# Three of the first four weight pieces loaded behind the first tile's inverse: a delta-rule attention with two feed-forward blocks on one core

## The reference

```
k_n = k / (norm(k) + 1e-6);  state = 0
for t in range(768):
    y[t]  = q[t] @ state
    state = state + beta[t] * outer(k_n[t], v[t] - state^T k_n[t])
```

```
x   = relu(x @ w_in)**2 @ w_out                      # 384 -> 2048 -> 384
out = max(x @ w1, x @ w2, x @ w3) @ w_out2           # 384 -> 768 -> 384
```

## Time and profile before

| what | value |
| --- | --- |
| median of 3 timed runs | 949.91 us (947.35 to 950.4) |
| the profiled execution's own time | 946.07 us |
| its span | 944.1 us |
| TensorE busy | 868.9 us, 92% of the span |
| VectorE, ScalarE, GpSimd busy | 45%, 28%, 30% |
| mean granted clock of TensorE | 0.969 of full speed |

### The profile page before, as it was taken

The page is one execution under the profiler, slowest core; times in us unless marked ns, Lnnn a source line. Parts: engine busy times, 40 slices in busy tenths (PEclk is TensorE's granted clock), DMA queues, the critical chain, the costliest instruction groups (busy, mean ns, idle before and its releaser), DMA issues.

```text
span 944.1 us, 20905 instructions
## 1 busy us (share of the span) xinstructions
PE 868.9 (92%) x9148; PEld 743.6 (79%) x9148; DVE 428.9 (45%) x641; ACT 265.8 (28%) x464; POOL 285.4 (30%) x392
## 2 busy tenths in 40 slices
PE   2326699999999999999999999999999999999998
PEld 2326588878888888888888888887898989898988
DVE  6936365574566456645544444434323232323231
ACT  2211343233223322332233233633222222122221
POOL 4147898813941394139400000721000000000000
PEclk8658899999999999999999999999999999999999
DMA  7976764165424532353223134012020202010000
GB/s 185 220 142 148 160 148 102 52 138 132 106 60 97 131 105 60 93 129 80 64 63 91 36 95 123 9 51 67 1 67 1 67 1 67 0 67 1 34 1 34
DMA packets 123435, 76.27 MB, mean 81 GB/s; under 512 B 94320, under 2 KB 107120, under 8 KB 123344
## 3 DMA queue, kind: packets, MB, share of 16 engines
q1 hardware_dynamic: 121088, 73.89, 31.7%
q10 hardware_dynamic: 2256, 1.05, 0.4%
HBM read 53.18 MB, written 20.45 MB: 78 GB/s over the span
## 4 chain that ended last, share of the span: by engine, by line
PE 89%; DMA 3%; DVE 3%; SPq 3%; issue 1%; ACT 0%; ACTq 0%; DVEq 0%
PE psum L71 25%; PE psum L73 24%; PE psum L72 24%; PE psum L667 3%; PE psum L605 2%; PE psum L591 2%; PE psum L616 2%; PE psum L655 2%; PE psum L674 2%; PE psum L631 1%; PE psum L642 1%; DMA dram_f<-sol_f 1%; SPq L372 1%; DMA kz_first<-in_kT 1%; SPq L326 1%
## 5 line engine op out<-in xcount | busy, mean ns | idle before, releaser
L967 DVE TENSOR_TENSOR sq<-relu 128x512 f32<-128x512 f32 x96 | 76.2, 793 | 151.2 <-ACT relu L1103 151.1
L73 PE MATMUL psum<-x_lo,wb 128*128 128x512 f32 x324 | 126.3, 390 | 0.0
L72 PE MATMUL psum<-x_hi,wb 128*128 128x512 f32 x324 | 126.3, 390 | 0.0
L71 PE MATMUL psum<-x_hi,wb 128*128 128x512 f32 x324 | 126.2, 389 | 0.0
L71 PE MATMUL psum<-x_hi,win 128*128 128x512 f32 x288 | 116.3, 404 | 9.0 <-DVE x_lo L956 7.9
L1103 ACT ACTIVATE relu<-psum 128x512 f32<-128x512 f32 x96 | 57.3, 597 | 228.6 <-PE psum L73 228.6
L104 POOL TENSOR_TENSOR sol_tmp<-sol_b,sol_f 128x31 f32<-128x31 f32 (+15 forms) x155 | 90.1, 581 | 84.6 <-DMA sol_b<-dram_b 72.7
L71 PE MATMUL psum<-sq_hi,wout 128*128 128x512 f32 x288 | 114.2, 396 | 1.0 <-DVE sq_lo L972 1.0
L72 PE MATMUL psum<-x_hi,win 128*128 128x512 f32 x288 | 113.2, 393 | 0.0
L73 PE MATMUL psum<-x_lo,win 128*128 128x512 f32 x288 | 113.1, 393 | 0.0
L73 PE MATMUL psum<-sq_lo,wout 128*128 128x512 f32 x288 | 112.4, 390 | 0.0
(11 more groups left out here) (99 smaller groups left out, 1280.0 us busy)
## 6 DMA issues: line engine op xcount, KB each, us to landing
kz<-in_kT SPq DMA_DIRECT2D x40, 192.0 KB, 3.5
v_t<-in_vn SPq DMA_DIRECT2D x12, 384.0 KB, 3.5
qa<-in_qT SPq DMA_DIRECT2D x24, 192.0 KB, 3.8
nz<-in_kn SPq DMA_DIRECT2D x24, 192.0 KB, 4.3
x2T<-x SPq DMA_DIRECT2D x6, 768.0 KB, 4.1
x_raw<-x2T SPq DMA_DIRECT2D x6, 768.0 KB, 4.6
out_dram<-o_t SPq DMA_DIRECT2D x24, 192.0 KB, 1.9
raw_wb<-in_w SPq DMA_DIRECT2D x18, 192.0 KB, 4.4
```

Source lines behind the costliest of these rows:

```text
L71: nc.tensor.matmul(out, lhs_hi, rhs_hi, start=first, stop=False)
L72: nc.tensor.matmul(out, lhs_lo, rhs_hi, start=False, stop=False)
L73: return nc.tensor.matmul(out, lhs_hi, rhs_lo, start=False, stop=last)
L967: nc.vector.tensor_tensor(d.sq[:], d.relu[:], d.relu[:], ALU.mult).then_inc(s.sq_ready, 1)
```

## The change

In SyncE's list the loads of piece 1 and piece 2, which stood right behind that of piece 0, now stand behind the store of tile 0's inverse and the loads of f1 and fz of chunk 0. The load of piece 4, with its wait for the fourth Gram product (kk_done), moves from ahead of that store to behind the loads of pieces 1 and 2. Piece 0 stays.

```
@@ -412,20 +412,20 @@
             sp.wait_ge(s.nz_zero, 1)
             load_kn(0)
             load_piece(0)
-            load_piece(1)
-            load_piece(2)
             sp.wait_ge(s.qk_done, 1)
             load_k(1, True)
             load_v(1)
             sp.dma_start(rows_of[2][:], kn[2]).then_inc(s.rows_in2, 16)
             sp.wait_ge(s.ob_zero, 3)
             load_ob(0)
-            sp.wait_ge(s.kk_done, 4)
-            load_piece(4)
             sp.wait_ge(s.fz_zero, 1)
             store_f(0)
             load_f1(0)
             load_fz(0, [1])
+            load_piece(1)
+            load_piece(2)
+            sp.wait_ge(s.kk_done, 4)
+            load_piece(4)
             for c in (2, 3):
                 sp.wait_ge(s.cg_ready, c + 1)
                 store_blocks(c, BLOCKS, s.b_stored)
```

## The result

The changed kernel took 953.88 us (median of 16 runs, 951.59 to 955.46), the one before 949.70 (16 runs, 945.15 to 952.12). The ratio is 1.005 with a 95% interval of 1.0035 to 1.0064: 3.3 to 6.1 us slower. A second comparison gave 953.40 against 950.23, ratio 1.0034 (1.0017 to 1.005), 3.2 us slower. The forecast was 953.8 and slower.

The account below looks back on a forecast made before the run. Until 104.3 us a chain of waits through the inverse's store and tile 1's root was taken as the bound, then TensorE. Root +3.6 and held norms +0.3 gave +3.9 on the 949.91 median: 953.8 us, range 949.1 to 957.2.

Parts of the forecast that it names:

- the text's own signs of being wrong: Root below 60.5, first dense matmul not moved as far as the root, or end not as far as that matmul.
- The store, the pieces and the root: Tile 1's root on ScalarE: store lands at 48.6, piece 2 is split at 61.0, root at 61.9 instead of 58.33, +3.6 us.
- the two cases: Piece 2 landing behind piece 1: 3.9 us in one earlier pair of loads, 4.9 in another; the middle, 4.4, was taken.
- VectorE beside GpSimd: Tile 1's norms held by GpSimd's low halves of piece 2, one or two meetings: +0.3 us, bounds -0.6 and +1.9.
- The cover: GpSimd's low halves, clearing sol_f, piece 4's issue and ScalarE's fz loads would be hidden under other waits, costing nothing.
- Pieces at peak rate: Rival: piece 2 lands 2.1 us behind piece 1, root at 59.6, sum +1.6, 951.5 us, no difference; chance 0.18.
- Piece 4 in the way of piece 2: Rival: piece 4's loads interleave with piece 2, landing up to 4 us later; root 65.9, +7.9, 957.8 us; chance 0.13.
- The faster side: Rival: the inverse's store sets the chain, so the root comes up to 8.8 us earlier; 941.1 us; chance 0.05.

Follow-up runs that it names:

- the kernel in which GpSimd waits: Changed kernel, with GpSimd waiting for the norms of tile 1 before making the low half of piece 2; 951.61 against 951.19 us before, ratio 1.0009.
- the kernels with the root first: Changed kernel, with ScalarE taking fz loads and tile 1's root before splitting pieces 1 and 2: 0.9944; splits later still: 0.9961; piece 4 also behind piece 3: 0.9924.

## Why the prediction was right, and where only by luck

The path was right: the root of tile 1 is released by the later of the store and the split of piece 2, the store came forward, piece 2 went back, and the start of the dense layer moved. The sizes were not. The total, +3.9 against +4.2 in the medians, is a sum of two terms that were both off, in opposite directions, and that it fits is luck. One of the text's own signs of being wrong came true: the root stands at 60.22, below 60.5. Nor did the first dense matmul move as far as the root, as forecast, but much further: by 8.1 us in the first profiles while the root moved by 1.9, and against the second profile of before, from the inverse's end, by about 6 and 0.6. Some of this did not reach the end: from the first dense matmul to the end of the span it took 839.8 and 840.8 us before and 838.7 and 840.0 now, a difference within the scatter of the profiles.

*The store, the pieces and the root: +3.6 forecast, +1.9 measured* (60.22 against 58.33; from the inverse's end 16.5 against 14.8 and 15.9, so +1.7 and +0.6). dram_f landed at 47.8, not 48.6, since its store took 3.6 us and not 4.5: 0.8. Piece 1 landed in 5.0 instead of 5.4 us: 0.4. Piece 2 was split 4.9 us behind piece 1, the upper of the two cases and not the middle: -0.5. The last 1.0 was an error of reading: 58.33 - 57.37 was counted as time that ScalarE needs for the two fz loads, but these are issued beside its activations (58.65 to 59.5 under the split that ends at 60.3). They had stood alone on the path only because ScalarE was idle. Together 1.7. What was forecast as nearly the whole loss was the smaller part: the kernel in which GpSimd waits has the root just as late (16.4) and is 0.9 us above before (-0.6 to +2.3).

*VectorE beside GpSimd: +0.3 forecast, +2.7 measured, beyond the stated bound of 1.9.* The bound allowed for one or two meetings; there were three, and one of them with the clearing of sol_f (L79, 1.89 us), which the text put at 63.6 without asking whether the norms were over by then. Now 0.62, 1.00 and 1.62 us were lost on L837, L838 and L839, against 0.58 on L835 before. The rule on two-input operations stood in the text beside the number and would have put the term at its upper end. It also said that the trace has one such meeting; it has two more, in the norms of the next tile:

```profile
84.84 0.63 DVE L838 TENSOR_TENSOR ssq<-ssq,norm_all 128x32 f32<-128x32 f32 x1
86.34 0.53 DVE L842 TENSOR_TENSOR c_all<-beta_all,c_all 128x32 f32<-128x32 f32 x1
```

GpSimd's operations beside them ran for 0.60 us from 84.83 and for 0.59 us from 86.23, and each of the two ended 0.04 to 0.05 us behind GpSimd's. So before the change the trace showed that one norms pass can meet several holds. The kernel in which GpSimd waits shows that this term is the larger part of the slowdown, with the reserve said there.

*The cover.* The low halves (as GpSimd's own work), the fz loads of ScalarE (issued at 58.65, used at 70.4) and piece 4's issue (part of the 3.84 us from 49.23) were hidden as forecast. One thing was not: the stretch from cg_first to the second L631 became 1.3 to 2.2 us longer in the two profiles. It did not in the kernel in which GpSimd waits, with the same order of loads. Its cause stays open. So does that of TensorE's granted clock in the last product ahead of the dense layer (L667): 1.00 of full speed (2.4 GHz) granted in both profiles of before, 0.50 (1.2 GHz) and 0.66 in those of the changed kernel, after the same wait of 2.69 us for VectorE. Columns as in the earlier trace rows, before and then changed:

```profile
93.50:98.50 5.00, 3.52 (x128) 3.40 (x128) 0.78 (x1) 1.08 (x2) 4.53 (x7) 1.00 0.11 40
```

```profile
99.80:104.80 5.00, 4.07 (x80) 4.07 (x82) 0.87 (x1) 0.34 (x1) 4.53 (x7) 0.50 0.15 52
```

That product took 2.09 us at the one and 3.69 at the other, and the stretch from the second L631 to the dense layer 28.2 us in both profiles of before and 29.6 and 29.4 in those of the changed kernel. Whether the change caused this is not shown: among the other eight kernels it was slow in six, without relation to their times.

*The rivals.* Pieces at peak rate: no, 4.9 us lay between the pieces. Piece 4 in the way of piece 2: not by the 4 us named, and within the bound of 4.9; 3.75 us between the pieces where piece 4 does not follow make it likely that it cost about 1 us. The faster side: the condition named there (ScalarE free when the store lands) is what the kernels with the root first create, and they are 4 to 7 us faster. With the same list of loads as the changed kernel, the first of them is 5.3 us below before: the loss hung on what stood ahead of the root on ScalarE and beside the norms on GpSimd.

## What to carry to other kernels

A load that is moved behind something is moved for every instruction that stands behind its user too: here a square root of 0.2 us stood behind the split of a weight piece that nobody needed for another 50 us. Of a moved piece of work on GpSimd, list each operation on VectorE with two SBUF inputs, and each tensor_scalar, that it will now run beside, and take one whole GpSimd operation for each of them as the upper bound; the tensor_scalar was the costliest here. And split a change into its parts before judging it: the half with the sign one wanted (piece 4 out of the store's way, 3.7 us) was there, hidden under the other.

## What the runs showed of the hardware

A two-input VectorE operation of 0.19 us was stretched to as much as 1.19 and 1.44 us, and a tensor_scalar of 0.18 to 1.80, each ending 0.03 to 0.05 us behind the end of a GpSimd operation; reciprocals between them kept their 0.35. Store issues on SyncE behind 2.3 MB of loads took 9.8 and 11.4 us for six, 6.7 behind 1.5 MB and 3.6 behind an empty queue. The second of two 512 KB stores issued together landed in 3.6 us when no weight piece had been loaded ahead of it since piece 0, in 9.8 behind the loads of the kernel before, in 8.6 with only piece 4 taken out of these and in 8.2 with only pieces 1 and 2 taken out.
